# Causal masks of an attention stage: divided by chunks over both heads, where they were divided by heads

## The reference

```python
# q, k, v, alpha: (4, 8, 768, 48) = batch, heads, sequence, head size
state = np.zeros((B, H, D, D), dtype=np.float32)
for t in range(S):
    state = alpha[:, :, t, :, None] * state + np.einsum('bhd,bhe->bhde', k[:, :, t], v[:, :, t])
    y[:, :, t] = np.einsum('bhd,bhde->bhe', q[:, :, t], state)
```

## Time and profile before

| | |
|---|---|
| median of three runs | 789.23 us (788.93 to 790.38) |
| the profiled execution | 790.78 us, span 789.0 us |
| TensorE busy in the span | 742.8 us (94%) |
| VectorE busy | 380.7 us (48%) |
| ScalarE busy | 273.4 us (35%) |
| GpSimd busy | 295.6 us (37%) |
| mean granted TensorE clock | 0.986 of full |

### The profile page before, as it was taken

The page is one execution under the profiler, slowest core; times in us unless marked ns, Lnnn a source line. Parts: engine busy times, 40 slices in busy tenths (PEclk is TensorE's granted clock), DMA queues, the critical chain, the costliest instruction groups (busy, mean ns, idle before and its releaser), DMA issues.

```text
span 789.0 us, 15500 instructions
## 1 busy us (share of the span) xinstructions
PE 742.8 (94%) x4774; PEld 653.6 (83%) x4775; DVE 380.7 (48%) x708; ACT 273.4 (35%) x638; POOL 295.6 (37%) x226
## 2 busy tenths in 40 slices
PE   4999999995699999999999999999999999999995
PEld 3888888884489999999999897788888888888885
DVE  6788888965843343333334228433333333333321
ACT  6778878775122322222222221211111112112110
POOL 3343443300381845727357489113133131220011
PEclk9999999998699999999999999999999999999998
DMA  9967565602483344425160220101101011000001
GB/s 187 274 123 180 108 164 103 166 1 87 177 340 132 128 155 166 165 78 188 52 209 31 83 62 22 31 11 40 31 31 47 14 40 30 20 20 0 11 21 50
DMA packets 128790, 74.49 MB, mean 94 GB/s; under 512 B 103448, under 2 KB 122016, under 8 KB 128736
## 3 DMA queue, kind: packets, MB, share of 16 engines
q1 hardware_dynamic: 118624, 53.53, 25.3%
q0 software_dynamic: 4096, 10.24, 3.5%
q10 hardware_dynamic: 6016, 10.07, 3.4%
HBM read 59.03 MB, written 14.79 MB: 94 GB/s over the span
## 4 chain that ended last, share of the span: by engine, by line
PE 77%; issue 13%; DVE 5%; POOL 2%; ACT 1%; DVEq 0%; ACTq 0%; POOLq 0%
PE bank L1425 53%; PE bank L1224 4%; PE bank L1254 4%; PE bank L1461 3%; PE bank L1317 3%; PE bank L1306 3%; PE bank L1285 3%; PE bank L1298 2%; PE bank L1272 1%; DVE Sm L895 1%; PE bank L1411 1%; POOL out L529 1%; DVE mh L1195 1%; PE bank L1483 1%; DVE low1h L1045 1%
## 5 line engine op out<-in xcount | busy, mean ns | idle before, releaser
L489 POOL TENSOR_TENSOR wsp<-raw,wsp 128x1536 f32 x28 | 103.7, 3726 | 91.9 <-DVE wsp L1110 91.9
L1425 PE MATMUL bank<-yh,mh 128*128 128x512 f32 x324 | 128.2, 396 | 0.1
L1425 PE MATMUL bank<-yh,ml 128*128 128x512 f32 x324 | 126.5, 390 | 0.0
L529 POOL DMA_INDIRECT out<-oo,tok_t x24 | 24.2, 1009 | 204.2 <-DVE oo L1167 204.2
L1425 PE MATMUL bank<-yl,mh 128*128 128x512 f32 x324 | 91.4, 390 | 0.0
L1425 PE MATMUL bank<-wsp,xh 128*128 (+1 forms) x324 | 85.3, 398 | 3.7 <-issue 3.2
L1425 PE MATMUL bank<-wsp,hTh 128*128 x432 | 81.8, 340 | 0.0
L813 ACT CAST gh<-t 128x512 fp32r<-128x512 f32 x36 | 22.4, 621 | 155.2 <-DVE t L1178 155.2
L1425 PEld LDWEIGHTS bank<-wsp,hTh 128*128 128x128 f32 x432 | 73.9, 188 | 0.2 <-issue 0.2
L1425 PEld LDWEIGHTS bank<-wsp,xh 128*128 128x128 f32 x324 | 58.9, 188 | 15.9 <-issue 4.1
L1425 PEld LDWEIGHTS bank<-yl,mh 128*128 128x128 f32 x324 | 60.8, 188 | 12.9
(11 more groups left out here) (207 smaller groups left out, 1323.4 us busy)
## 6 DMA issues: line engine op xcount, KB each, us to landing
raw<-in_moe_w SPq DMA_DIRECT2D x16, 1536.0 KB, 7.9
expert_rows<-ye ACTq DMA_DIRECT2D x27, 193.0 KB, 2.9
yg<-expert_rows SPq DMA_DIRECT2D x24, 193.0 KB
nat<-in_alpha SPq DMA_DIRECT2D x32, 144.0 KB, 2.8
nat<-in_k SPq DMA_DIRECT2D x32, 144.0 KB, 3.0
nat<-in_q SPq DMA_DIRECT2D x32, 144.0 KB, 3.0
vt<-in_v SPq DMA_DIRECT2D x32, 144.0 KB, 3.0
attention_rows<-xc SPq DMA_DIRECT2D x4, 1152.0 KB, 5.3
```

The lines of the kernel that those rows point to most:

```text
L489: g.tensor_tensor(wsp[:, ds(to, 1), 1, n, part], raw[:, n:n + 1, part], wsp[:, ds(to, 1), 0, n, part].bitcast(f32), ALU.subtract).then_inc ...
L529: g.indirect_dma_start(out=out, out_offset=bass.IndirectOffsetOnAxis(ap=tok_t[:, i, 0:1], axis=0), in_=oo[i % 2][:], in_offset=None).then_ ...
L1425: last = mm(o, x, y, start=(n == 0), stop=(n == len(todo) - 1))
```

## The change

A mask instruction now covers both heads and a part of the chunks of its group: the first part two chunks (128 x 512 elements), the second part the one chunk that is left (128 x 256). For this the banks 6 and 7 become one PSUM tensor of two banks, and the mask operand is read once for each head with a stride of zero. Both parts wait until the scores of both heads are there. TensorE's value products of a group wait for the first part, and before the last chunk of the group (`cc == HC*h + HC - 1`) for the second. The counts of `dve_S` and of the instructions are the same: two masks for each group.

```diff
-    bank = [nc.alloc_psum_tensor(f"bank{i}", [P, 512], f32) for i in range(8)]
+    bank = [nc.alloc_psum_tensor(f"bank{i}", [P, 512], f32) for i in range(6)]
+    both = nc.alloc_psum_tensor("bank6_7", [P, 2, 512], f32)
+    bank += [both[:, n, :] for n in range(2)]
...
-        def mask(u, j, grp, hd):
+        def mask(u, j, grp, part):
 
             dve.wait_ge(pe_Y, CR + 2 * (u - 2) + 2)
-            dve.wait_ge(pe_S, 4 * u + 2 * grp + hd + 1)
-            d.tensor_tensor(Sm[j % 2][:, hd, HC * grp:HC * grp + HC, :], cols(bank[6 + hd], 0), causal[:],
+            dve.wait_ge(pe_S, 4 * u + 2 * grp + 2)
+            cs = (slice(0, HC - 1), slice(HC - 1, HC))[part]
+            n = (HC - 1, 1)[part]
+            got = both[:, :, 0:HC * P].rearrange("p h (c n) -> p h c n", c=HC)[:, :, cs, :]
+            keep = causal[:, cs, :].rearrange("p (o c) n -> p o c n", o=1).to_broadcast([P, 2, n, P])
+            d.tensor_tensor(Sm[j % 2][:, :, HC * grp:HC * grp + HC, :][:, :, cs, :], got, keep,
                             ALU.mult).then_inc(dve_S, 1)
...
-            for hd in range(2):
-                mask(u, j, 0, hd)
+            for part in range(2):
+                mask(u, j, 0, part)
             if base + j + 1 < NU:
                 scale_k(u + 1, nxt)
-            for hd in range(2):
-                mask(u, j, 1, hd)
+            for part in range(2):
+                mask(u, j, 1, part)
             states(u, j)
...
-                pe.wait_ge(dve_S, CR + 4 * u + 2 * h + 2)
+                pe.wait_ge(dve_S, CR + 4 * u + 2 * h + 1)
                 for cc in range(HC * h, HC * h + HC):
+                    if cc == HC * h + HC - 1:
+                        pe.wait_ge(dve_S, CR + 4 * u + 2 * h + 2)
                     for hd in range(2):
                         mm(out(cc)[HL * hd:HL * hd + HL], vt[j][:, cc, hd, :], Sm[j % 2][:, hd, cc, :],
                            start=(cc == HC * h), stop=(cc == 0), skip_group_check=True)
```

## The result

The changed kernel takes 794.14 us (median of 5 runs, 793.02 to 794.99) against 789.23: 1.0048 times the kernel before, interval 1.0032 to 1.0065. (The medians alone would give 1.0062, which also lies in the interval.) It is slower by 2.5 to 5.1 us, where no change was forecast (789.4, range 788.1 to 791.2). The five executions of either kernel lie within 2 us of each other; larger sets of the kernel before, beside the experiments, scatter over 3 to 5.5 us. A part of the scatter is a gap of some 2 us early in the feed-forward layer, which 8 of the 13 traces have (those of both kernels among them) and 5 have not. The profiled execution took 794.89 us, its span is 793.1; that is 4.1 above the profiled one of before.

A forecast was written before the change was run, and what follows sets the result against it. The chain from V to the last UA was taken to bound each attention unit. The moved wait gains 0; (0.006 + 0.004) us x (16 + 4) = 0.2 us on 789.23 gives 789.4 us, range 788.1 to 791.2.

The forecast's parts named there:

- What bounds the kernel: Attention units: TensorE is early for the last carry and waits for the last UA; its loads start 0.11 to 0.12 us later.
- The wait moved forward: gain 0: Group 1's value products start 0.32 us earlier, but the last carry still waits for the last UA, so nothing is gained.
- Rival A: Attention units: carries follow value products freely, so each unit gains 0.30 us, 4.8 us in all, giving 784.4 us; chance 0.07.
- Size of the masks: VectorE's masks in attention: the two parts take 690 + 417 = 1107 ns, where the two halves took 1106.
- jumps in the pattern: VectorE's mask operands, now two runs each: 0 to 8 ns more a group, taken as 4.
- rival B: VectorE's masks: reading over two PSUM banks costs a fresh start each, 0.13 us a group, giving 792.2 us; chance 0.11.
- Score wait: First mask of each group: waiting for both heads' scores starts it 0 to 0.01 us later, taken as 0.006.

The follow-up runs named there:

- e5: The changed masks alone, with TensorE waiting for both parts before a group's value products as in the kernel before: 1.0010 times the kernel before.
- e1: The kernel before with four idle instructions in TensorE's program just ahead of the routing's wait for r_hot, masks untouched: 1.0054 times the kernel before.
- e8: The changed kernel with sixteen idle instructions in the branch of TensorE's program that never runs: 1.0033 times the kernel before.
- e12: The changed kernel with 252 idle instructions in the branch of TensorE's program that never runs: 1.0022 times the kernel before.
- e2: The changed kernel with eight idle instructions in TensorE's program just ahead of the routing's wait for r_hot: 1.0065 times the kernel before.

## Why the prediction was wrong, step by step

*What bounds the kernel* was right. The wait for the last UA is the one that decides: with idle time ahead of the value products (before, e5) and without it (the changed kernel), the last carry's loads stand 0.11 behind the last UA in all sixteen units, and the units differ only by when V starts.

*The wait moved forward: gain 0* was right, and so was the picture of it: idle time gone, TensorE's busy time up (749.0 against 742.8 us, 6.2 where I had said 3 to 5), last loads still 0.11 behind the last UA. Rival A, which would have been read off the chain of waits, was wrong by its whole 4.8 us.

*Size of the masks* and *jumps in the pattern*: 692 and 414 ns against my 690 and 417 plus 4. Jumps between long runs cost nothing here (the two parts take 1106 ns, the two halves took 1106), which agrees with the page of the Trainium skill that the prediction names; and rival B's price for the read over two banks (0.13 us a group) is nothing: V comes 0.94 behind the first mask as before.

*Score wait* was the right term with a wrong size: 0.006 us a group were taken from the modelled ends of two matmuls, and it is 0.042 in the loop units. It makes 0.7 us of the loss. I priced when the results are there and not when the second increment arrives.

**The step that failed** is one that isn't in the sum. The change was taken with the same counts of `dve_S` and of instructions, which is so for VectorE's masks, and its only effect on TensorE's program as a wait. That the new wait's value has to be computed in the loop, by four register instructions (15512 instructions against 15500), was put at nothing without a reason. What they cost is not their own time but their place: they lie ahead of the routing in TensorE's text, and the second routing matmul stands for 2.0 us in the changed kernel's trace. That place alone does it: four idle instructions on the kernel before are 1.0054 (e1), and without the four (e5) the gap is gone and 1.0010 is left. Rival B had the sign, and its 792.2 lies nearer to the measured 794.14 than my 789.4, but for a reason that isn't there; that is luck.

What stays open: with the gap taken away, 1.0033 (e8) and 1.0022 (e12) remain, where the masks alone give 1.0010 (e5). The traces don't put this on the change. When the expert layer is nearly done (at 470 us in the trace of before) all three are equally late, by 1.2 to 1.3 us: the 0.7 of the masks and what each happens to lose or win before unit 1, in the third unit and in the routing's low clock. What parts them afterwards (spans of 790.4, 788.6 and 788.2 us) is the gap early in the feed-forward layer, which e8 has and e12 and e5 have not. It is in the waits of before, 472 to 500 us:

```profile
PEld bank L1483 <- issue: 1.9, 1, 1.9
```

The times of e12 fall in groups 2 us apart (three at 790.3 to 790.5, most at 792.2 to 792.9), as those of the kernel before on the same chip do (eight at 789.1 to 789.5, most at 790.5 to 792.3). Low group against low group e12 is some 1.2 us slower. So a median also depends on how many executions have such a gap or stall. Only one execution of each kernel has a trace, so how often the gap comes, why it comes, and whether the change makes it more frequent isn't shown.

## What to carry to other kernels

When two waits end one after the other in a loop, only the later one has a price; find it by a constant distance between a producer's end and the consumer's loads over several units, since drawn busy time hides it. Move what heads that chain (V here) before moving what fills the idle time. And count an edit's instructions in each engine's program text: where a jump has work waiting behind it, four more instructions can cost more than the edit's whole effect. Idle instructions placed in the part that is jumped over show it, and took the gap away here.

## What the runs showed of the hardware

- Instructions come in pieces by DMA: 26 pieces with 0.43 MB in one queue (16 KB each), 28 with 0.23 MB in another (8 KB). After the jump over the stepwise way, the text behind the next boundary came 4.7 us after the branch's end in the changed kernel, 5.6 in e1 and 5.7 in e2, where TensorE had reached the boundary by 192.3 us and stood until 197.3. Where sixteen or 252 instructions more were jumped over, the branch itself took 3.5 to 3.7 us instead of 1.1 to 1.9. The Trainium skill, "Advanced Engine Details and Errata", section "ISA Cache", gives a cache line of 16 KB, 256 instructions. The first queue agrees; the 8 KB pieces of the second are not in it.
- A wait for the second of two increments from matmuls that start together ended 0.042 us later than a wait for the first; raised by two at once, 0.016 (loop units).
- A wait that had become a VectorE instruction of its own made its mask start 0.07 later than one that was part of the mask (0.12 against 0.05).
- One read of VectorE over two PSUM banks cost the same as two reads of one bank with as many elements (692 + 414 against 2 x 553 ns).
